# Block-ordering transfers of a fused attention and two-MLP kernel split over two issuing queues, with attention blocks, staging steps and additions re-placed

## The reference

```python
scores = scale * np.matmul(q_c, k_c.transpose(0, 1, 2, 4, 3))   # q, k, v: 4 x 8 heads x 576 x 64, chunks of 64
attn = np.exp(scores - max) ; attn = attn / (sum + 1e-09)        # within each chunk
x = (attn @ v_c), heads side by side                             # 2304 tokens x 512
h = x @ w_in;  x = (h - np.tanh(h)) @ w_out                      # first MLP, 512 -> 2048 -> 512
h = x @ w_in2; out = (h * np.tanh(softplus(h))) @ w_out2         # second MLP, same sizes
```

## Time and profile before

| what | us |
|---|---|
| timed runs, median of 2 | 905.52 |
| profiled execution, its own time | 898.54 |
| its span | 896.8 |
| TensorE busy | 821.9 |
| VectorE busy | 616.2 |
| ScalarE busy | 376.6 |
| GpSimd busy | 184.2 |

### The profile page before, as it was taken

One profiled execution on the slowest core, in us unless ns is written; L12 is line 12 of the kernel. 1 busy time (PEld: TensorE's weight loads), 2 busy tenths in 40 slices (PEclk: granted clock), 3 DMA queues, 4 the chain that ended last, 5 costly groups with the idle time before them and its releaser, 6 DMA issues. The chain is left out here.

```text
span 896.8 us, 13616 instructions
## 1 busy us (share of the span) xinstructions
PE 821.9 (92%) x5298; PEld 749.6 (84%) x5298; DVE 616.2 (69%) x871; ACT 376.6 (42%) x539; POOL 184.2 (21%) x227
## 2 busy tenths in 40 slices
PE   7999667867778889989999999999999999999998
PEld 7999666867777778979989979898888989888896
DVE  6776634637767665747666578888877777777775
ACT  4444322323333333424443355544645344453543
POOL 3331223321533324305533000212000000000000
PEclk9999988989999999989999999999999999999999
DMA  7553334651545535648888943548734239442401
GB/s 248 187 180 116 105 106 143 212 189 48 187 177 188 188 130 200 221 173 313 325 315 322 367 157 118 181 171 302 308 141 158 89 114 378 153 165 83 154 12 71
DMA packets 50816, 165.80 MB, mean 185 GB/s; under 512 B 8000, under 2 KB 11840, under 8 KB 50752
## 3 DMA queue, kind: packets, MB, share of 16 engines
q1 hardware_dynamic: 40896, 129.26, 39.0%
q0 software_dynamic: 9856, 35.66, 11.8%
HBM read 110.36 MB, written 50.59 MB: 179 GB/s over the span
## 5 line engine op out<-in xcount | busy, mean ns | idle before, releaser
L1535 PE MATMUL psum<-w_lo,w_hi 128*128 128x384 f32 x288 | 97.6, 339 | 0.0
L1536 PE MATMUL psum<-w_hi,w_lo 128*128 128x384 f32 x288 | 97.1, 337 | 0.0
L1534 PE MATMUL psum<-w_hi 128*128 128x384 f32 x288 | 96.4, 335 | 0.7 <-DVE pool_words L1190 0.7
L1419 PE MATMUL psum<-w_hi 128*128 128x384 f32 x192 | 67.1, 350 | 13.9 <-DVE pool_words L1065 4.1
L1555 PE MATMUL psum<-w_hi,g_lo 128*128 128x512 f32 x192 | 76.1, 396 | 0.0
L1554 PE MATMUL psum<-w_lo,g_hi 128*128 128x512 f32 x192 | 75.9, 395 | 0.0
L1553 PE MATMUL psum<-w_hi,g_hi 128*128 128x512 f32 x192 | 74.9, 390 | 0.5 <-DVE pool_words L1005 0.4
L1357 PE MATMUL psum<-g_hi,w_hi 128*128 128x384 f32 x128 | 46.6, 364 | 30.2 <-DMA pool_words<-pool_words 30.2
L845 ACT ACTIVATE pool_words<-pool_words 128x768 f32<-128x768 f32 x48 | 40.3, 839 | 77.2 <-DVE pool_words L1158 77.2
L1162 DVE SCALAR_TENSOR_TENSOR pool_words<-pool_words 128x768 f32<-128x768 f32 x48 | 51.7, 1078 | 21.9 <-ACT pool_words L845 21.9
L1420 PE MATMUL psum<-w_lo,w_hi 128*128 128x384 f32 x192 | 66.2, 345 | 0.0
(11 more groups left out here) (173 smaller groups left out, 2232.9 us busy)
## 6 DMA issues: line engine op xcount, KB each, us to landing
w_hi<-s_hi SPq DMA_DIRECT2D x32, 896.0 KB, 5.0
w_lo<-s_lo SPq DMA_DIRECT2D x32, 896.0 KB, 7.3
pool_words<-w POOLq DMA_DIRECT2D x32, 256.0 KB, 3.5
pool_words<-w_out POOLq DMA_DIRECT2D x32, 256.0 KB, 4.2
s_hi<-w_hi SPq DMA_DIRECT2D x8, 896.0 KB, 5.5
s_lo<-w_lo SPq DMA_DIRECT2D x8, 896.0 KB, 7.3
w_hi<-t_hi SPq DMA_DIRECT2D x18, 384.0 KB, 5.5
w_lo<-t_lo SPq DMA_DIRECT2D x18, 384.0 KB, 6.6
```

The lines of the kernel that those rows point to most:

```text
L1419: pe.matmul(ps, a_hi, t_hi_words[:, k, :], start=first, stop=False, skip_group_check=i in (M5, M3))
L1534: pe.matmul(ps, a_hi, t_hi_words[:, k, :], start=first, stop=False, skip_group_check=i in (M5, M3))
L1535: pe.matmul(ps, a_hi, t_lo_words[:, k, :], start=False, stop=False, skip_group_check=i in (M5, M3))
L1536: mm = pe.matmul(ps, a_lo, t_hi_words[:, k, :], start=False, stop=end, skip_group_check=i in (M5, M3))
```

## The change

1. Blocks 6 to 17: of the eight ordering transfers of a block, SyncE issues the four of chunk 0 and GpSimd the four of chunk 1, at places in its list given by `ORDERED_AHEAD_OF`; TensorE waits for both counts.
2. Group 1: blocks 9, 10 and 11 move from F tiles 9, 12 and 14 to 10, 13 and 15. The y1 of an F tile now stands ahead of the wait for the block, and the outputs run 3 behind up to tile 10, none at tiles 2 and 11, and 4 behind from tile 12. y1 of tiles 12, 13 and 14 run behind the loop, y1 of tile 15 behind place 5 of pair 0.
3. The end of group 1: `keep_x(11)`, the first two splits of the tokens and the shift and exps of block 12 move behind the loop. `keep_x(11)` waits for the scores of block 12 and no longer for its shift, and the shift waits for `keep_x(11)`.
4. Pairs: the steps of pairs 1 to 6 move one slot earlier. On VectorE u3 goes ahead of slot 1, c21 and c22 ahead of slot 2 (the transposes between them), and c12 ahead of the subtraction of the tanh. Beside a block, six slices of output work stand ahead of the wait for the block, and two behind it.

```diff
-LAST_LAG = 4
+OUTPUT_BEHIND = {f: f - 3 if f < 11 else f - 4 for f in range(3, FT) if f != 11}
...
-BLOCK_AT = {(0, 6): 3, (0, 10): 4, (0, 14): 5, (1, 1): 6, (1, 4): 7, (1, 7): 8, (1, 9): 9, (1, 12): 10, (1, 14): 11}
+BLOCK_AT = {(0, 6): 3, (0, 10): 4, (0, 14): 5, (1, 1): 6, (1, 4): 7, (1, 7): 8, (1, 10): 9, (1, 13): 10, (1, 15): 11}
...
-STEPS_BESIDE_BLOCK = (1, 1, 0, 0, 1, 1, 1)
+STEPS_BESIDE_BLOCK = (1, 1, 1, 1, 0, 1, 1)
...
-    if _q == 2:
-        place_steps([(_q, 0)], _T[0][3:4])
-    place_steps([(_q, 1)], _d[0:1])
-    if _q in (1, 3, 4):
-        place_steps([(_q, 2)], [_T[0][{1: 2, 3: 5, 4: 6}[_q]]])
-    place_steps([(_q, 3), (_q, "w1")], _d[1:3])
+    place_steps([(_q, 0)], _d[0:1])
+    if _q < 5:
+        place_steps([(_q, 1)], [_T[0][{1: 2, 2: 3, 3: 5, 4: 6}[_q]]])
+    place_steps([(_q, 2), (_q, 3)], _d[1:3])
...
+ORDERED_AHEAD_OF = {}
+for _t, _at in ((6, ("group", 1)), (7, ("group", 2)), (8, ("group", 5)), (9, ("group", 8)), (10, ("group", 11)),
+                (13, (1, 2)), (14, (3, 2)), (15, (4, 2)), (16, (5, 2)), (17, (6, 2))):
+    ORDERED_AHEAD_OF.setdefault(STEP_AT[_at][0], []).append(_t)
+ORDERED_AHEAD_OF.setdefault(STEP_INDEX["direct", 2, 0], []).append(11)
@@ GpSimd @@
+            def order_blocks(t):
+                pool.wait_ge(blocks_turned, t - GROUP_TILES + 1)
+                for q1 in range(2):
+                    for k1 in range(2):
+                        to, at = block_move(1, q1, k1)
+                        pool.dma_start(to, at).then_inc(blocks_ordered_pool, 16)
...
             for k in range(EARLY_STEPS):
+                for t in ORDERED_AHEAD_OF.get(k, ()):
+                    order_blocks(t)
                 if k == STEP_INDEX["direct", 2, 0]:
                     add_x(0)
+                    order_blocks(12)
                     add_tokens(0, 2)
@@ SyncE, order_blocks @@
-                for c in range(2):
+                for c in range(2 if t < 2 * GROUP_TILES else 1):
@@ ScalarE, keep_x @@
-                if t < TILES - 1:
+                if t == 11:
+                    act.wait_ge(scores_ready, t + 2)
+                elif t < TILES - 1:
                     act.wait_ge(shifted, t + 2)
...
-                    if g == 1 and f == FT - 1:
-                        x1_hi(0, 0)
-                        x1_hi(0, 1)
...
                 mlp1_group(g)
+            keep_x(11)
+            x1_hi(0, 0)
+            x1_hi(0, 1)
+            exps(12)
@@ VectorE, shift @@
+                if t == 12:
+                    dve.wait_ge(x_next_done, 9)
@@ VectorE, mlp1_pair @@
+                take1_u3(q)
                 beside_pair_lo(q, 1)
-                take1_u3(q)
+                if q == PAIRS + 1:
+                    keep_wide_y(0)
+                take1_c21(q)
                 if scored < TILES:
                     turn_blocks(scored)
-                if q == PAIRS + 1:
-                    keep_wide_y(0)
+                take1_c22(q)
                 beside_pair_lo(q, 2)
-                take1_c21(q)
                 beside_pair_lo(q, 3)
-                take1_c22(q)
+                take1_c12(q)
+                minus1(2 * q)
                 beside_pair_lo(q, "w1")
-                minus1(2 * q)
-                take1_c12(q)
                 lo1(2 * q)
@@ VectorE, behind the groups @@
+            x1_lo(0, 0)
+            x1_lo(0, 1)
+            shift(12)
...
@@ TensorE, mlp1_group @@
-                lag = LAST_LAG if g == PLAIN - 1 else LAG1
                 for f in range(1, FT):
                     hidden(g, f)
...
-                    if (g, f) in BLOCK_AT:
+                    if g == 0 and (g, f) in BLOCK_AT:
                         wait_for_values(BLOCK_AT[g, f])
                         wait_for_scores(BLOCK_AT[g, f] + 1)
-                    if f >= lag:
-                        y1(g, f - lag)
-                    elif f < LAG1 and g > 0:
-                        y1(g - 1, FT + f - LAG1)
+                    if g == 0 and f >= LAG1:
+                        y1(g, f - LAG1)
+                    if g == 1 and f < LAG1:
+                        y1(0, FT + f - LAG1)
+                    if g == 1 and f in OUTPUT_BEHIND:
+                        y1(g, OUTPUT_BEHIND[f])
...
                     if (g, f) in BLOCK_AT:
+                        if g == 1:
+                            wait_for_values(BLOCK_AT[g, f])
+                            wait_for_scores(BLOCK_AT[g, f] + 1)
                         values(BLOCK_AT[g, f])
                         scores(BLOCK_AT[g, f] + 1)
...
-                        y1(PLAIN - 1, FT - 2)
+                        y1(PLAIN - 1, FT - 1)
...
-                if q == 0:
-                    y1(PLAIN - 1, FT - 1)
...
-            y1(PLAIN - 1, FT - 4)
-            y1(PLAIN - 1, FT - 3)
+            for f in range(FT - 4, FT - 1):
+                y1(PLAIN - 1, f)
```

More of the change, by code:

```diff
@@ L270, in token_block, with block_move @@
             return y_block(s, t, k)
+        def block_move(c, q1, k1):
+            rows, to_rows = (slice(c * CHUNK + 32 * h, c * CHUNK + 32 * h + 32) for h in (q1, k1))
+            return ordered_words[to_rows, q1 * 256:(q1 + 1) * 256], turned_blocks[rows, k1, :, :].rearrange("p h q -> p (h q)")
         def x_block(w, t, k):
@@ L328, in build @@
         norm_steps, probs_ready = sem("norm_steps"), sem("probs_ready")
-        blocks_turned, blocks_ordered = sem("blocks_turned"), sem("blocks_ordered")
+        blocks_turned, blocks_ordered, blocks_ordered_pool = sem("blocks_turned"), sem("blocks_ordered"), sem("blocks_ordered_pool")
         turned, turned_copied, values_ready, x_next_done = sem("turned"), sem("turned_copied"), sem("values_ready"), sem("x_next_done")
@@ L507, in order_blocks @@
                 sp.wait_ge(blocks_turned, t - GROUP_TILES + 1)
-                for c in range(2):
+                for c in range(2 if t < 2 * GROUP_TILES else 1):
                     for q1 in range(2):
                         for k1 in range(2):
-                            rows, to_rows = (slice(c * CHUNK + 32 * h, c * CHUNK + 32 * h + 32) for h in (q1, k1))
-                            sp.dma_start(ordered_words[to_rows, q1 * 256:(q1 + 1) * 256],
-                                         turned_blocks[rows, k1, :, :].rearrange("p h q -> p (h q)")).then_inc(blocks_ordered, 16)
+                            to, at = block_move(c, q1, k1)
+                            sp.dma_start(to, at).then_inc(blocks_ordered, 16)
             def wait_for_stores(k):
@@ L1026, in mlp1_group @@
                         split_x_lo()
-                    if g == 1 and f == FT - 1:
-                        x1_lo(0, 0)
-                        x1_lo(0, 1)
                     minus_tanh(n)
-                    if scores_of is not None and scores_of < 12:
+                    if scores_of is not None:
                         normalise(scores_of)
@@ L1291, in wait_for_values @@
                 else:
-                    pe.wait_ge(blocks_ordered, 128 * (t - GROUP_TILES + 1))
+                    if t < 2 * GROUP_TILES:
+                        pe.wait_ge(blocks_ordered, 128 * (t - GROUP_TILES + 1))
+                    else:
+                        pe.wait_ge(blocks_ordered, 128 * GROUP_TILES + 64 * (t - 2 * GROUP_TILES + 1))
+                        pe.wait_ge(blocks_ordered_pool, 64 * (t - 2 * GROUP_TILES + 1))
                 if t in (1, 2):
```

## The result

The changed kernel took 879.51 and 880.64 us, median 880.08, against 905.52 before: ratio 0.972, 95% interval 0.969 to 0.975. That is 25 us less, where 46 were forecast, and outside the range of 849 to 876. Measured again with more runs it took 877.43 us against 907.36, ratio 0.968 (0.964 to 0.972).

What follows compares the result with a forecast made beforehand. TensorE was taken to bound the kernel, losing time ahead of pair 7 by waiting, not by load. Savings of 31.0 + 0.9 + 11 + 3 = 45.9 us off 905.5 gave 859.6 us, range 849 to 876.

Steps and rivals of the forecast that it cites:

- term 5: Pair 9: its 2.2 us wait at place 6 goes, with part of the clock; 3 us saved.
- term 2: Group 1: 30.2 us of y1's waits for ordering transfers and some clock removed, less 5.6; 31.0 us saved.
- S + 10: A block's ordering is done 10 us after its scores end (S), against S + 12.4 before.
- term 4: Pairs 2 to 6: 108.3 us laid out anew as 94.5, four fifths of the 13.8 counted; 11 us saved.
- Term 1: Ordering transfers: GpSimd's half lands about 2 us after issue, so a block is in order at S + 10.
- signs of being wrong: Wrong if GpSimd's issues took over 1 us or landed after over 4, or hidden waited for VectorE in group 1.
- 873 us: Rival: GpSimd's half lands as late as all eight did, order at S + 12.4; about 873; chance 0.14.
- the staging steps become the bound: Rival in group 1: three stalls of 3 to 4 us at staging steps, and their clock; about 872; chance 0.09.
- Term 3: End of group 1 with pair 0, −0.5 us, and pair 1, −0.4; together 0.9 us saved.
- the layout of pair 2: Pair 2 laid out anew, place 6 no longer waiting; 20.8 us with a late subtraction and its clock kept.

Runs made afterwards that it cites:

- split_only: The kernel before with only the ordering transfers split over SyncE and GpSimd; old places, lags and VectorE order; ratio to the kernel before 0.985.
- step_later: The changed kernel with weight job 1's three staging steps one F tile later in group 1 (11, 12, 13); ratio to the kernel before 0.964.
- slot_later: The changed kernel with SyncE's 1.8 MB store of slot 0 behind the ordering of block 11 instead of ahead; ratio to the kernel before 0.963.
- all_sp: The changed kernel with all eight ordering transfers issued by SyncE again, none by GpSimd; ratio to the kernel before 0.991.
- pairs_old: The changed kernel with steps, VectorE's order and output slices of all pairs as before; split and group 1 stay changed; ratio to the kernel before 0.972.
- late_old: The changed kernel with VectorE's old order in pairs 8 to 15 only; ratio to the kernel before 0.966.
- combo_old: The changed kernel with three corrections, the edits of slot_later, step_later and late_old together; 862.1 us, ratio to the kernel before 0.951.
- combo_end: combo_old with weight job 1's last two parts at F tiles 14 and 15, GpSimd's half of block 11 ahead of them; ratio to the kernel before 0.951.
- steps_first: The changed kernel with slots 2 and 3 ahead of c21 and c22 again in pairs 8 to 15; ratio to the kernel before 0.964.
- w1_first: The changed kernel with VectorE's slot w1 ahead of the subtraction of tanh again in pairs 8 to 15; ratio to the kernel before 0.966.
- after_again: The changed kernel, no edit, traced a second time; ratio to the kernel before 0.968.

## Why the prediction was wrong

Of the 26.4 us that are missing in the trace, 13.9 are term 5 (the new order costed only in pair 9), 6.6 term 2 (one chain, S + 10, for all blocks) and 4.8 term 4 (the raw weights of pair 2 taken as landed, and the split as costing nothing there); 1.2 lie ahead of group 1. The mechanism of the split and of the cover was right.

**Term 1, the split: right, but for block 11.** GpSimd's price, taken as about 2 us from below the 2.7 to 7.8 of its larger transfers, was 1.7 to 1.8 where nothing was in the way, and an issue 0.50 us. For block 11 its transfers landed after 4.8 to 5.2 us, one of the signs of being wrong that I had named. The Trainium skill's rule ("DMA: Bandwidth & Descriptors", "SWDGE vs HWDGE vs iDMA") that GpSimd's descriptors can be shut out by VectorE didn't show: 48 issues took 0.498 to 0.532 us, most of them beside VectorE's next step. That section ties the rule to a "2-port perf mode" of VectorE, a condition that my prediction left out; without having checked it I shouldn't have said that the rule makes 873 us the forecast. No run shows in which mode these steps ran, so they are no test of it. `split_only` measured about what the step said, in part by luck (blocks 7 and 11).

**Term 2, group 1: the mechanism right, the size wrong** (31.0 forecast, 24.4 measured). The step that failed is "S + 10", a chain of one length for all blocks. It held for blocks 7 to 9. For block 10 a staging step stood ahead of shift and exps, and hidden waited 2.5 us and values(10) 1.4, with some 1.6 for the clock: I had this as a rival ("the staging steps become the bound", 0.09) and priced it with three stalls, but it doesn't replace the forecast, it adds to it. Hidden waiting for VectorE was also one of the signs of being wrong that I had named. `step_later` removed it. For block 11 I took 3.4 us and 1.7 for the clock against `keep_slot(0)`; it was 5.2 and about 2.4, and `slot_later` showed that it goes with this store. Waits and clock came to 13.1 us, where I had 5.6. The deeper fault: beside y1's waits ScalarE had waited for additions unseen (2.6, 3.3 and 4.6 us in group 1 before), and I asked only whether the engines had the capacity (51 us of 76), not whether each step's transfer would land before the step.

**Term 3, pairs 0 and 1: right in size** (0.9 forecast, 1.0 measured), with the 4 us wait for u2 in pair 1 that its working contains. That it agrees to 0.1 us is luck, since pair 0 alone took 13.1 to 16.9 us with the same code. values(12) came 23.9 us earlier, not 32, for what group 1 lacked.

**Term 4, pairs 2 to 6: half** (11 forecast, 6.2 measured; over traces with each order and the split, pairs 1 to 6 took 119.6 to 127.0 us with the new one, 129.1 and 131.2 with the old). c22 no longer holds up place 6, as forecast. The step that failed is the layout of pair 2: it assumes that the raw weights of the step at slot 0, which stands ahead of u2, are there. They hadn't landed:

```profile
221.75 0.84 ACT L756 ACTIVATE w_hi<-pool_words 128x768 fp32r<-128x768 f32 x1 [4.98 <-DMA pool_words<-w]
```

What made them late is the split, which I had put at nothing here ("GpSimd's four issues fall in its idle time, except in pair 3"). GpSimd's loads now stand behind its part of block 13's ordering, and SyncE, done with its own part sooner, issues a store of 1.8 MB at 212.3 us, ahead of the loads at 213.0. `all_sp` shows it: the order of the pairs is the new one and SyncE does all the ordering, so the loads (223.9 us) stand ahead of that store (226.8); ScalarE has the weights 5.3 us after the first load's issue, not 8.7, TensorE doesn't wait for u2, and pair 2 takes 19.9 us. With the split and the old order it is 23.9 and 24.3 us (`pairs_old`, `split_only`); in the changed kernel it was 24.1 in both traces, where I had 20.8. Pair 3 took 22.9 and 19.9 us (forecast 20.0), pair 4 19.2 and 20.8 (18.2); their excess changes from trace to trace and isn't traced to a step. The layout for pairs 5 and 6 was right to 0.3 us (18.3 and 17.6 us against 18.2 and 17.3).

**Term 5, pair 9: the step right, its neighbours overlooked** (3 forecast, −10.9 measured for pairs 7 to 15). Place 6 of pair 9 doesn't wait any more, and the pair is 4.1 us shorter. But I had costed the new order only where the old one waited. In pairs 10 to 14 next to nothing waited before (1.4 us, in pairs 12 and 13), so I read nothing there, while the same edit moves every pair's steps behind c22 and the w1 split behind the subtraction. These free buffers, and GpSimd's list loads behind them: in this stage the 16 engines are 0.71 busy (0.75 before), a load takes up to 10 us, and the two issued 2.9 and 2.3 us later than before are late for place 4 of pairs 12 and 13. The order is what does it: seven traces with the old one (both of the kernel before, `split_only`, `pairs_old`, `late_old`, `combo_old`, `combo_end`) took 136.6 to 140.8 us for pairs 8 to 15, five with the new one (both of the changed kernel, `slot_later`, `step_later`, `all_sp`) 142.8 to 148.0. This is the largest single error: 10.9 us in the first trace, some 7 between the means of the two sets. Of the waits for u2 more is due to the steps than to slot w1: `steps_first` took them from 8.0 to 3.0 us and issued one load earlier, `w1_first` left the loads where they were. Pairs 8 and 10 have other waits, told above.

**The basis.** The first trace before was a short execution, 7 us under the median; the second was 10 us longer. This didn't decide the miss: the first traces of the two kernels differ by 19.5 us, the second ones by 34, the medians by 25 to 30.

With the three corrections the kernel reached 862.1 us, near the 859.6 forecast. That is 45 us under the median of the kernel before beside it. But stage by stage against the first trace before it is 35.1: 29.2 of the 31.0 in group 1, 1.1 in pairs 0 and 1, 4.5 of the 11 in pairs 2 to 6 and 0.5 of the 3 behind them. So group 1 held nearly what was forecast, the pairs didn't, and the near agreement of the times is in part the short trace that the prediction started from.

## What to carry to other kernels

When a wait of the bounding engine goes, list what the other engines waited for under its cover, with the transfer behind each, and lay these out too; whether the engines have the capacity doesn't answer it, the order of their lists does. When an edit changes a loop body, cost it in every pass, above all where nothing waits now and the transfer engines are nearly full, and follow each moved step to the load that it releases. Keep bulk stores behind small urgent transfers in a queue, not ahead of them, and when a queue is shortened, look what bulk transfer moves up with it.

## What the runs showed of the hardware

- GpSimd issued a transfer of 32 rows of 1 KB in 0.50 us and it landed in 1.7 to 1.8 us; SyncE took 0.59 and 1.8 to 2.2 for the same (block 11 of `slot_later`). I had taken 0.56 and about 2 for GpSimd.
- With a store of 1.8 MB issued 6 us earlier, the same transfers took 4.8 to 5.7 us from the two queues (5.1 to 5.9 and 4.2 to 5.2 in `after_again` and `late_old`); without it 1.7 to 2.2, though GpSimd's own stores and loads of similar size had been issued 6 to 10 us before. In the kernel before, with all eight from SyncE, it was 2.4 to 4.4 us behind that store.
- The kernel before, the same work each time, varied from 902.1 to 911.7 us between executions, with a mean granted clock from 0.972 down to 0.961. Where two traces were laid side by side, half of their difference of 10 us was one late transfer and what followed.
